# Attention and a gated MLP in one kernel: the batch loop of every engine written out in sequence

## What is computed

```python
q_rot, k_rot = rotate(q), rotate(k)                     # x1*cos - x2*sin, x1*sin + x2*cos
scores = matmul(q_rot, k_rot.T) / sqrt(64)
attn = exp(scores - max(scores)); attn = attn / (sum(attn) + 1e-9)
x = matmul(attn, v)                                      # 4 x 576 x 512, heads side by side
h = maximum(x @ w_in, 0)                                 # 4 x 576 x 1024
conv_out = sum(conv_w[k] * shifted(h, k - 1) for k in range(3))
y = (h * sigmoid(conv_out)) @ w_out                      # 4 x 576 x 512
```

## Time and profile before

| what | value |
|---|---|
| median of 3 runs | 574.83 us (572.93 to 576.76) |
| profiled execution, device time | 577.52 us |
| its span, first to last instruction | 575.7 us |
| mean granted TensorE clock | 0.917 of full |
| TensorE matmul busy | 456.1 us, 79% |
| TensorE weight load busy | 407.9 us, 71% |
| VectorE busy | 419.3 us, 73% |
| ScalarE busy | 280.5 us, 49% |
| GpSimd busy | 202.7 us, 35% |

### The profile page before, as it was taken

How to read it: one execution, slowest core, us unless ns; L and a number is a source line. 1 busy time by engine, 2 the same in 40 slices (tenths; PEclk the granted TensorE clock), 3 DMA queues, 4 the chain that set the end, 5 groups by cost and what they waited for, 6 DMA issues and landing times.

```text
span 575.7 us, 17377 instructions
## 1 busy us (share of the span) xinstructions
PE 456.1 (79%) x6784; PEld 407.9 (71%) x6784; DVE 419.3 (73%) x796; ACT 280.5 (49%) x655; POOL 202.7 (35%) x277
## 2 busy tenths in 40 slices
PE   0045777859998699869998699869998698869996
PEld 0034656758998577659998477658998476659996
DVE  6978487727997987837997987836997979845441
ACT  1232555515766453525766453425666445425542
POOL 5312577522331254422331254421431244421221
PEclk9999979779999597979999597889999789889999
DMA  6888322025567011225567011224567102200011
GB/s 205 232 246 248 143 84 84 3 85 202 150 194 183 15 47 42 84 88 193 158 177 189 27 37 51 83 89 170 167 175 181 52 2 85 84 4 1 2 42 42
DMA packets 24368, 62.56 MB, mean 109 GB/s; under 512 B 3296, under 2 KB 7392, under 8 KB 21984
## 3 DMA queue, kind: packets, MB, share of 16 engines
q1 hardware_dynamic: 24288, 61.43, 34.3%
HBM read 42.55 MB, written 4.72 MB: 82 GB/s over the span
## 4 chain that ended last, share of the span: by engine, by line
PE 51%; DVE 18%; issue 12%; DMA 7%; POOL 4%; ACT 4%; SPq 2%; DVEq 0%; POOLq 0%; ACTq 0%
PE banks L366 15%; PE banks L338 6%; DVE neg_max L607 5%; PE banks L398 4%; PE banks L400 4%; PE banks L399 4%; PE banks L382 4%; PE banks L384 4%; PE banks L383 4%; DVE turned L632 3%; PE banks L339 3%; DVE conv L643 3%; DMA Q<-K 2%; DMA xs<-qk_swapped_dram 2%; DVE xs L592 2%
## 5 line engine op out<-in xcount | busy, mean ns | idle before, releaser
L472 ACT ACTIVATE P<-banks,neg_max 128x576 f32<-128x576 f32 x144 | 106.8, 742 | 134.3 <-DVE neg_max L607 133.2
L338 PE MATMUL banks<-K,Q 128*128 128x288 f32 x256 | 98.0, 393 | 76.1 <-ACT P L472 42.1
L607 DVE TENSOR_REDUCE neg_max<-banks 128x1 f32<-128x576 f32 x144 | 106.5, 742 | 42.0 <-PE banks L339 33.6
L338 PEld LDWEIGHTS banks<-K,Q 128*128 128x128 f32 x256 | 58.3, 228 | 104.6 <-ACT P L472 56.8
L761 POOL TENSOR_SCALAR P<-P,recip 128x576 f32<-128x576 f32 x124 | 91.9, 752 | 103.3 <-DVE recip L624 103.3
L366 PE MATMUL banks<-turned,V 32*64 32x128 f32 (+1 forms) x4608 | 109.9, 322 | 21.6 <-DVE turned L632 20.4
L765 POOL TENSOR_TENSOR u_lo<-u,u_hi 128x288 fp32r<-128x288 f32 x64 | 61.9, 968 | 173.8 <-ACT u_hi L505 173.8
L366 PEld LDWEIGHTS banks<-turned,V 32*64 32x64 f32 x4608 | 90.3, 146 | 33.9 <-issue 29.2
L632 DVE STREAM_TRANSPOSE turned<-P 128x576 f32<-128x576 f32 x144 | 109.0, 761 | 3.2 <-PE banks L366 3.1
L643 DVE SCALAR_TENSOR_TENSOR conv<-banks,taps,conv 128x288 f32<-128x288 f32 x128 | 65.8, 514 | 37.7 <-ACT conv L494 37.4
L339 PE MATMUL banks<-KL,Q 128*128 128x288 f32 x256 | 84.3, 340 | 0.0
(11 more groups left out here) (50 smaller groups left out, 620.2 us busy)
## 6 DMA issues: line engine op xcount, KB each, us to landing
V<-v_rows_dram SPq DMA_DIRECT2D x16, 1152.0 KB, 5.1
xc<-qk_dram SPq DMA_DIRECT2D x28, 288.0 KB, 2.9
xs<-qk_swapped_dram SPq DMA_DIRECT2D x28, 288.0 KB, 4.2
KL<-Q SPq DMA_DIRECT2D x32, 144.0 KB, 3.8
Q<-K SPq DMA_DIRECT2D x32, 144.0 KB, 3.6
K<-K SPq DMA_DIRECT2D x32, 144.0 KB, 3.0
y_dram<-y_sb SPq DMA_DIRECT2D x8, 576.0 KB, 3.3
wi_raw<-w_in_dram SPq DMA_DIRECT2D x1, 2048.0 KB, 8.0
```

The source lines that it names most:

```text
L338: nc.tensor.matmul(out, Q[:, h, qc], K[:, h, cols], start=True, stop=False)
L472: nc.scalar.activation(dst, src, ACT.Exp, bias=neg_max[:, c:c + 1], scale=1.0, accum_out=row_sum[:, c:c + 1]).then_inc(exps, 1)
L607: nc.vector.tensor_reduce(out=neg_max[:, c:c + 1], in_=banks[:, 2 * (t % 2):2 * (t % 2) + 2, 0:HALF], axis=AX.XY, op=ALU.max, negate=True) ...
```

## The change

The five hardware loops become Python loops that run when the program is built. The instructions of the three iterations are written out one behind the other on each engine, b is a number, and every count in a wait is a constant. Order, tiles, buffers, semaphores and the work of each engine stay as they were; registers, register arithmetic and branches of the loops go.

```diff
@@ sync
-            with sp.Fori(0, B - 1) as b:
+            for b in range(B - 1):
                 batch(b, False)
             batch(B - 1, True)
@@ tensor
-            with pe.Fori(0, B - 1) as b:
+            for b in range(B - 1):
                 last_values(b)
                 gated_mlp(b, False)
                 attention(b + 1)
@@ scalar
-            with act.Fori(0, B - 1) as b:
+            for b in range(B - 1):
                 x_high(b, PAIRS - 1)
                 gated_mlp(b, False)
                 attention(b + 1, False)
@@ vector
-            with dve.Fori(0, B - 1) as b:
+            for b in range(B - 1):
                 x_low(b, PAIRS - 1)
                 gated_mlp(b, False)
                 attention(b + 1)
@@ gpsimd
-            with pool.Fori(0, B - 1) as b:
+            for b in range(B - 1):
                 gated_mlp(b, False)
                 attention(b + 1, False)
```

## The result

The kernel with everything written out takes 581.02 us (576.57 to 585.54, 20 executions) against 576.93 us (572.93 to 580.98, 20 executions) for the kernel before: a ratio of 1.0074, from 1.0044 to 1.0103. It is slower by about 4 us. The profiled execution took 580.93 us, with a span of 579.1 us; before it was 577.52 and 575.7.

What follows compares the result with a forecast made beforehand. Waits between engines, in stages, were taken to bound the kernel, with no engine full. Branches 0, registers 0, tail tiles +0.6, last values -0.6 and pauses 0 summed to 0: 574.8 us, range 571.8 to 578.5.

Steps and rivals of the forecast that it cites:

- What bounds the kernel: Whole kernel: no engine is full, waits between engines set the time in stages; in the MLP TensorE's matmuls fill it.
- Pauses in straight code: TensorE's loads in the last values: three pauses of about 0.7 us would shift; no change taken, bounds -2.1 and +3.5 us.
- Branches: Loop ends: removing TensorE's two taken branches, 3.68 and 3.30 us, gains 0, as TensorE waits there anyway; bound 7.0 us.
- Register arithmetic: Waits of score tiles and maxima in attention: register operations, 7.4 us together, run while engines are busy; removing them gains 0.
- Tail tiles: Attention's 12 tail tiles in three later batches: late wait on its own instruction, 0.6 us slower; bounds 0 and 1.2 us.
- Last values: Small matmuls behind attention's last turned tile: three batches start 0.2 us sooner each, 0.6 us gained; bounds 0 and 0.8 us.
- The other signs named beforehand: Changed profile: MLP windows with 85 matmuls in 11 us, and an instruction queue of 54 to 57 packets.
- code arrives too late: Products with V: 13 more pauses of 0.7 us in the long straight program, +9.1 us, 583.9 us; chance 4%.

Runs made afterwards that it cites:

- with V moved: Changed kernel, with SyncE issuing the next batch's V load behind the first four rotary loads instead of ahead; 1.0033 of the kernel before at first, 1.0040 in the final table.
- loop shifted by 80: Kernel before, hardware loops kept, plus 80 instructions only incrementing an unused semaphore ahead of TensorE's first wait; 586.1 us against 576.55, ratio 1.0161.
- with the load out of the way: Kernel before with only TensorE's loop written out and the V load issued behind the first rotary loads; ratio 1.0002 to the kernel before.

## Why the prediction was wrong

It said 574.8 us (571.8 to 578.5), with 0.88 for within 1%. The ratio, +0.74%, is within 1%, but the time, 581.0 us, lies outside the range. 2 us of the distance are the level: the kernel before has a median of 576.93 over 20 executions, not the 574.83 of three. Of the other 4 us, 2.3 are a missing term, TensorE's (0.40%); 1.7 belong to the other three engines, and 1 of these stays open. (A slip of 0.1 us beside that: the range's lower end should be 574.8 - 2.9 = 571.9.) Step by step:

- **What bounds the kernel: the failing step.** "In the MLP the matmuls of TensorE fill the time" was read from 11 us in the middle of the stage. Its start is another matter: one load that lands between 0.15 us ahead of its use and just late, in each of the three batches, in front of VectorE, in front of a full TensorE. I never asked for the slack of the loads, as SyncE's issues stayed where they were.
- **Pauses in straight code, and the same failing step.** I had the moving packet ends, took them for pauses of TensorE's own, and bounded them by -2.1 and +3.5 us. The pauses in fact went the good way: the three of 0.68, 0.78 and 0.67 us inside the last values have become one of 0.15 us (0.79 us in the repeat of the same kernel and 1.51 us with V moved, so the length varies). What I left out is that a packet uses the DMA engines beside the loads. The term was +2.3 us (0.40% from TensorE alone), and most of 9 us in a loop shifted by 80.
- **Branches: 0, right for this kernel.** The taken branches of 3.7 and 3.3 us are gone and nothing came of it: TensorE alone written out, with the load out of the way, takes 1.0002. The slack of 1.0 us was thin: in the loop shifted by 80 the branches took 5.06 us and the last values started 0.7 us behind their tile. The rule of the Trainium skill ("Runtime: NRT & Kernel Launch", Instruction fetch mechanics) that a taken branch stalls for its target's code agrees with the stall in the earlier trace rows; the time of 567.8 us by it is 13 us from the measured one, and the 7.0 us of stalls didn't come back, because TensorE was waiting there anyway. That code fetch is mostly hidden, as the same section says, doesn't hold for this kernel shifted by 80: the fetches cost up to 9 us (586.1 against 576.55), most of it through somebody else's load.
- **Register arithmetic: 0, right.** From tile 5's maximum to tile 9's it takes 196.62 - 188.94 = 7.68 us in batch 1, as in the earlier trace rows; batch 2's 8.11 us are the wait for the store.
- **Tail tiles: +0.6, right in kind, a little less.** The list for line 333, idle time ended by what (us, times), now has 16 of each kind, as foretold:

```profile
  issue: 18.3, 16
  ACT P L472: 14.5, 16
```

  All 12 first loads now start 0.11 us behind the sum instead of 0.05. But only the tiles 4 and 13 show it in the maxima, 0.07 us each; at tiles 22 and 31 the spacing stays 1.55. That is 0.4 us.
- **Last values: -0.6, right.** The changed kernel's timeline for batches 0 to 3:

```profile
121.01 7.12 PEld L366 LDWEIGHTS banks<-turned,V 32*64 32x64 f32 x282 [6.94 <-DVE turned L632]
...
250.86 7.12 PEld L366 LDWEIGHTS banks<-turned,V 32*64 32x64 f32 x288 [4.63 <-DVE turned L632]
...
383.83 6.87 PEld L366 LDWEIGHTS banks<-turned,V 32*64 32x64 f32 x266 [4.63 <-DVE turned L632]
390.85 0.47 PEld L366 LDWEIGHTS banks<-turned,V 32*64 32x64 f32 x22 [0.15 <-issue]
...
514.69 6.81 PEld L366 LDWEIGHTS banks<-turned,V 32*64 32x64 f32 x288 [4.63 <-DVE turned L632]
```

  They start 0.05 us behind the turned tile in all four batches, where three had 0.23, 0.27 and 0.22. That is the start only; the whole stage changed by +0.12, -0.90, +0.17 and -0.31 us.
- **The other signs named beforehand:** the full middle of the MLP stayed, 85 matmuls in 11 us in all four batches; the instruction queue has 53 packets and not 54 to 57.
- **Not in the sum at all:** VectorE's own late wait (0.3 us) and its 0.36 us in batch 3. I had looked for two-wait places only on TensorE.
- **The rival "code arrives too late"** (583.9 us, 4%) had the right suspect and the wrong victim: it expected more pauses in TensorE's loads, and there were not more.

No version clearly beats the kernel before; the nearest, SyncE alone written out, is at 0.9978 with an interval that reaches 1.0009.

## What to carry to other kernels

An edit that only changes how many instructions an engine has also changes when its code is fetched, and the fetches share the DMA engines with the data. So before trusting "same work, same order", look in the trace for loads that land within a few tenths of a us of their use at the start of a full stage; they are what such an edit breaks, and a large transfer queued ahead of a small urgent one is the thing to move. Padding one engine's program with idle instructions ahead of its first work is a cheap test of how exposed a kernel is. And where one instruction has two waits, see which of them comes last on every engine, not on the bottleneck alone.

## What the runs showed of the hardware that was not expected

- A single 16 KB packet of code (of 53 to 59 in the whole run) went with a landing about 1.4 us later for a 288 KB load queued behind 1152 KB (7.02 instead of 5.62 us), and about 2.1 us later for a store of 576 KB (5.5 instead of 3.4). Spread over 16 engines, at the 335 GB/s that moved between the load's issue and its landing, 16 KB would be 0.05 us. But the packet takes 0.9 us of one engine (0.8% of 16 over 7.02 us), and one engine is then the last to finish, alone for 1.3 us. The trace doesn't say whether it is the same one. Where the 0.4 us between the two comes from, and the rest of the store's 2.1, was not found.
- 1.4 us of wait at the start of the MLP cost 3 us: TensorE's idle time of 2.08 us was followed by matmuls spaced at 0.24 instead of 0.14 us until 272 us, at the lower clock level (granted clock 0.50 from 269.20 to 272.50 us).
- The taken branches of 3.3 and 3.7 us cost nothing behind a wait that lasts longer. How long one takes depends on where the code lies: 80 instructions more ahead of the loop made it 5.06 us, twice.
